# Large SBUF buffers placed at multiples of 2048 bytes in a float32 scan and feed-forward kernel

## The reference, cut to what matters

```python
# x, f_logit: (2, 6080, 256), all float32
sig = 1.0 / (1.0 + np.exp(-f_logit))
f = lower_bound + (1.0 - lower_bound) * sig
i = 1.0 - f
for t in range(S):                      # a gated running sum over 6080 steps
    h = f[:, t] * h + i[:, t] * x[:, t]
    y[:, t] = h
# then per token, d_model 256, d_ff 2048
h = y @ w_in
g = h * np.clip(h + 3.0, 0.0, 6.0) / 6.0
out = g @ w_out
```

## The kernel before, in words

| buffers | before | after |
|---|---|---|
| w_in_raw, w_out_raw, w_in_hi, w_in_lo, w_out_hi, w_out_lo | 128 | 0 |
| x_sb, z_sb, sig, gate, drive, state | 1280 | 0 |
| state_hi, state_lo, clipped, g, g_hi, g_lo, y_sb | 1312 | 0 |
| warm (1024 bytes) | 256 | 0 |

## Time and profile before

### The profile page before, as it was taken

How to read it: one execution, slowest core, us unless ns; L and a number is a source line. 1 busy time by engine, 2 the same in 40 slices (tenths; PEclk the granted TensorE clock), 3 DMA queues, 4 the chain that set the end, 5 groups by cost and what they waited for, 6 DMA issues and landing times.

```text
span 1083.2 us, 12791 instructions
## 1 busy us (share of the span) xinstructions
PE 1074.5 (99%) x4636; PEld 873.8 (81%) x4636; DVE 621.4 (57%) x950; ACT 533.2 (49%) x859; POOL 70.9 (7%) x37
## 2 busy tenths in 40 slices
PE   7999999999999999999999999999999999999998
PEld 7998888888888888888888888888888888888886
DVE  7865564655646556465564655646556465564644
ACT  5655454454544545444454444544445445454443
POOL 3300000000000000000000000000000000000000
PEclk9999999999999999999999999999999999999999
DMA  7011010110101101011010110101101001010000
GB/s 262 1 56 56 1 59 0 58 58 0 58 6 52 58 0 58 13 46 58 0 58 17 41 58 0 58 21 37 58 0 58 24 34 58 0 58 20 1 20 19
DMA packets 22093, 41.74 MB, mean 39 GB/s; under 512 B 1600, under 2 KB 3136, under 8 KB 22080
## 3 DMA queue, kind: packets, MB, share of 16 engines
q1 hardware_dynamic: 22080, 41.56, 11.4%
HBM read 29.10 MB, written 12.45 MB: 38 GB/s over the span
## 4 chain that ended last, share of the span: by engine, by line
PE 98%; DVE 0%; ACT 0%; issue 0%; ACTq 0%
PE y_ps L465 49%; PE h_ps L445 49%; DVE state L349 0%; DVE state_lo L379 0%; ACT clipped L263 0%; DVE g_lo L364 0%; DVE g L359 0%; DVE drive L342 0%; ACT y_sb L324 0%; ACT state_hi L277 0%; ACT g_hi L268 0%; ACTq L262 0%
## 5 line engine op out<-in xcount | busy, mean ns | idle before, releaser
L263 ACT ACTIVATE clipped<-h_ps,half 128x512 f32<-128x512 f32 (+1 forms) x384 | 263.2, 686 | 533.6 <-PE h_ps L445 533.6
L359 DVE SCALAR_TENSOR_TENSOR g<-clipped,h_ps 128x512 f32<-128x512 f32 (+1 forms) x384 | 261.7, 682 | 450.2 <-ACT clipped L263 450.1
L445 PE MATMUL h_ps<-state_hi,w_in_hi 128*128 128x512 f32 (+1 forms) x768 | 303.2, 395 | 3.3 <-DVE state_lo L379 3.3
L465 PE MATMUL y_ps<-g_hi,w_out_hi 128*128 128x512 f32 (+1 forms) x768 | 302.5, 394 | 1.0 <-DVE g_lo L364 1.0
L445 PE MATMUL h_ps<-state_lo,w_in_hi 128*128 128x512 f32 (+1 forms) x768 | 302.8, 394 | 0.0
L445 PE MATMUL h_ps<-state_hi,w_in_lo 128*128 128x512 f32 (+1 forms) x768 | 302.7, 394 | 0.0
L465 PE MATMUL y_ps<-g_lo,w_out_hi 128*128 128x512 f32 (+1 forms) x768 | 302.3, 394 | 0.0
L465 PE MATMUL y_ps<-g_hi,w_out_lo 128*128 128x512 f32 (+1 forms) x768 | 302.3, 394 | 0.0
L364 DVE TENSOR_TENSOR g_lo<-g,g_hi 128x512 fp32r<-128x512 f32 (+1 forms) x384 | 271.2, 706 | 0.2
L268 ACT CAST g_hi<-g 128x512 fp32r<-128x512 f32 (+1 forms) x384 | 233.0, 607 | 1.6 <-DVE g L359 1.4
L445 PEld LDWEIGHTS h_ps<-state_hi,w_in_hi 128*128 128x128 f32 x768 | 144.9, 189 | 37.0 <-DVE state_lo L379 2.9
(11 more groups left out here) (23 smaller groups left out, 77.9 us busy)
## 6 DMA issues: line engine op xcount, KB each, us to landing
z_sb<-in_z SPq DMA_DIRECT2D x22, 512.0 KB, 4.5
x_sb<-in_x SPq DMA_DIRECT2D x22, 512.0 KB, 5.1
out_y<-y_sb SPq DMA_DIRECT2D x21, 512.0 KB, 3.3
w_in_raw<-in_w_in SPq DMA_DIRECT2D x8, 256.0 KB, 5.9
w_out_raw<-in_w_out SPq DMA_DIRECT2D x8, 256.0 KB, 7.1
out_y<-y_sb SPq DMA_DIRECT2D x2, 448.0 KB, 3.5
out_y<-y_sb SPq DMA_DIRECT2D x2, 256.0 KB, 2.1
z_sb<-in_z SPq DMA_DIRECT2D x2, 224.0 KB, 3.7
```

The source lines that it names most:

```text
L263: nc.scalar.activation(clipped[:, s, 0:n], h_ps[:, s, 0:n], ACT.Relu, bias=half[:], scale=1.0 / 6.0).then_inc(clipped_ready, 1)
L359: nc.vector.scalar_tensor_tensor(g[:, s, 0:n], clipped[:, s, 0:n], 1.0, h_ps[:, s, 0:n], ALU.min, ALU.mult).then_inc(g_ready, 1)
L445: last = nc.tensor.matmul(h_ps[:, s, 0:n], w[:, f, k, :], v[:, b, k, 0:n], start=(k == 0 and m == 0), stop=(k == K - 1 and m == len(terms) ...
L465: last = nc.tensor.matmul(y_ps[:, b, d, 0:n], w[:, f, at], v[:, s, 0:n], start=(f == 0 and m == 0), stop=(f == F - 1 and m == len(terms) - 1))
```

## The change

A filler of 1920 bytes is put ahead of the first buffer, so that it begins at byte 18432 = 9 x 2048. The small tensors (`lb_sb`, `one_minus_lb`, `lb_minus_one`, `half`, `warm`, `carry`), which lay between the large ones, are allocated behind all of them. Each large buffer is a multiple of 2048 bytes long, so all of them then begin at multiples of 2048. No instruction, operand shape, wait or transfer is changed, on any engine.

```diff
+ROW = 2048
+PAD_FROM = 16512
...
+        sb("pad", [P, ROW - PAD_FROM % ROW], mybir.dt.uint8)
         w_in_raw = sb("w_in_raw", [P, F, K, P])
         w_out_raw = sb("w_out_raw", [P, F, D])
         w_in_hi = sb("w_in_hi", [P, F, K, P], F32R)
         w_in_lo = sb("w_in_lo", [P, F, K, P], F32R)
         w_out_hi = sb("w_out_hi", [P, F, D], F32R)
         w_out_lo = sb("w_out_lo", [P, F, D], F32R)
-        lb_sb = sb("lb_sb", [P, K])
-        one_minus_lb = sb("one_minus_lb", [P, K])
-        lb_minus_one = sb("lb_minus_one", [P, K])
-        half = sb("half", [P, 1])
-        warm = sb("warm", [P, WARM_N], F32R)
...
         state = sb("state", [P, K, N])
-        carry = sb("carry", [P, B, K])
         state_hi = sb("state_hi", [P, B, K, N], F32R)
...
         y_sb = sb("y_sb", [P, B, K, N])
+
+        warm = sb("warm", [P, WARM_N], F32R)
+        lb_sb = sb("lb_sb", [P, K])
+        one_minus_lb = sb("one_minus_lb", [P, K])
+        lb_minus_one = sb("lb_minus_one", [P, K])
+        half = sb("half", [P, 1])
+        carry = sb("carry", [P, B, K])
```

## The result

The changed kernel takes 1053.73 us (median of 4 runs, 1052.91 to 1055.17) against 1084.74 (1084.52 to 1084.92) before: ratio 0.9713, 95% interval 0.9699 to 0.9727. The medians lie 31.0 us apart and the spans of the two profiled executions 30.0, since the profiled execution of the changed kernel was the slowest of its four runs: it took 1055.17 us for a span of 1053.2. So the time of a run lies 2.0 us above its own span there, not the 1.6 that the prediction adds; this shifts nothing in what follows.

A forecast was written before the change was run, and what follows sets the result against it. TensorE's matmul spacing bounds the kernel: 4224 x 0.2343 + 384 x 0.2000 = 1066.5 us, with opening and end a span of 1083.2. All change terms were zero; plus 1.6 gives 1084.8 us, range 1056 to 1088.

The forecast's parts named there:

- the 1.6 that the prediction adds: Whole run: the median run time lies 1.6 us above the profiled span, added to every predicted span.
- The unexplained step of 5.8 to 7.7 ns: 512-column matmuls: excess over the cost seen with 448 columns, 24.5 to 32.5 us if placement removed it.
- I take zero: Spacing of 512-column TensorE matmuls: the new placement changes nothing, 0 us, out of bounds up to 88.7 us.
- the term on weight loads: TensorE weight loads: 0.19 us each, hidden, ended 0.04 us before use, alike at four block starts; 0 us.
- The argument from alternating sizes: Mixed 448- and 512-column matmuls: the extra cost falls behind and catches up, so it is not tied to an address.
- The first had the right size: Rival on streamed rows: 512-column rows are cheaper within one 2048-byte stretch; 1060.3 to 1052.3 us, chance 0.27.
- The second named the right partners: Rival on stream and loads: everything at remainder 0 collides, slower; 1090 to 1106 us, chance 0.16.
- The short matmuls: 448-column matmuls on TensorE: expected to stay 200 ns apart.
- ACT, DVE, POOL: Operands of these engines move to remainder 0; 3.4 us of cover remain, so 0 us.
- Opening: Transfers at the start: first matmul within a microsecond of 9.44; plus or minus 0.5 us together with the final store.
- The 16-byte lines: SBUF rule: remainders 1312 and 0 both begin a 16-byte line, so the move is worth nothing.
- N / 2.4 + 2.5 ns: Matmul spacing rule: 215.8 ns for 512 columns; 78 us less should placement be the whole reason for the difference.

The follow-up runs named there:

- e3: Changed kernel with every large buffer at remainder 32 by 2048 instead of 0; 1053.7 us.
- e11: Changed kernel with the 448-column streamed rows written to and read from columns 40 to 487, 160 bytes in; median 1053.00 us, ratio 0.9690 to before.
- e8: Changed kernel with weights left at remainder 0 and every other large buffer at 32 by 2048; 1082.6 us.
- e5: Changed kernel with state rows at remainder 512 and g rows at 1024 by 2048, all else at 0; 1053.4 us.
- e10: Kernel before with only a 96-byte filler ahead of state_hi, so rows start at 1408 and weights stay at 128; 1054.4 us, ratio 0.9697.
- e4: Kernel before with only TensorE's operands (split weights and streamed rows) moved to remainder 0, other buffers as before; 1054.3 us.
- e1: Kernel before with only the weight buffers moved to remainder 0, streamed rows still at 1312; 1082.4 us.
- e6: Changed kernel with weights left at remainder 0 and every other large buffer at 256 by 2048; 1053.5 us.
- e7: Changed kernel with weights left at remainder 0 and every other large buffer at 64 by 2048; 1061.9 us.
- e2: Kernel before with only the streamed rows moved to remainder 0, weights still at 128; 1079.3 us.

## Why the prediction was wrong

The views were read rightly: TensorE alone is the bound, and the only lever of that size is the spacing of 512-column matmuls, 4.2 us for each nanosecond. The unexplained step of 5.8 to 7.7 ns was sized rightly too; 7.62 is what went. In part that is luck: the yardstick was the short matmuls' 13.3 ns beyond their columns, and they happened to lie at a place that is among the best for them. After the change they paid 20.0 ns, more than the long ones' 13.3.

*The step that failed* is "I take zero" for that spacing. It put at nothing a term of 7.62 ns for each matmul, 32.2 us. It rested on two arguments. The first, that the 448-column row from the same remainder 1312 paid only 13.3 ns, was about the row's own place, and as such its conclusion holds: e3 has a row off every multiple of 64 and across a multiple of 2048, at no cost. But it was taken to clear every address, and from another length, while lengths don't share their best placement: at distance 160 the short ones are at their best (200.0, again in e11) and the long ones at their worst (234.3). The second, in the term on weight loads, was the decisive fault. I held that weight blocks started at 128, 640, 1152 and 1664 without a difference, so the place of the weights didn't matter. These four are one and the same place by 256 (remainder 128). The trace had no variation in the one quantity that counts, and I took its evenness for evidence that nothing counts. e3 against e8 shows it: the rows unmoved, the weights' place alone worth 6.7 ns.

*The argument from alternating sizes*, "a rate and not a penalty at an address", made a false choice: it is a rate, and the addresses have a part in it. Not the whole: the changed kernel has the lag as well, with all places alike. In its chain the groups of six long ones among short ones still take 1.40 us at 88.79, and 1.36 only from 99.42 on.

```profile
88.79 1.40 PE h_ps L449 x6
91.41 1.40 PE h_ps L449 x6
...
99.42 1.36 PE h_ps L449 x6
```

*The rivals.* The first had the right size, 1052.3 to 1060.3, and the wrong reason: not the multiple of 2048 (e3, e5, e10). I had its chance at 0.27, and the range cut it at 1056 where its upper price alone gave 1052.3. The second named the right partners, the stream and the load beside it, and had the sign the wrong way round: a common place by 256 is the free one. It said that meeting at the same remainder "is not new, save for the load", which was the thing to follow up.

*The short matmuls* were forecast at 200 and came at 206.7 in that profile, 2.6 us against the gain. *Weight loads hidden*: right as to the wait and wrong as to the cost, since the place of a block whose load is hidden still changes the spacing. *ACT, DVE, POOL*: right, e4 moved them alone and nothing came of it. *Opening*: right, 9.06 for 9.44; over all profiles here it began between 8.5 and 9.6 us.

The Trainium skill (TensorE: Matmul & The Clock Gate, Step-by-step: what each phase is for) says that loading the next weights takes no read bandwidth from the running matmul. These runs speak against it for float32r: with the rows unmoved, the weights' place is worth 6.7 ns of every matmul (e3, e8). The 16-byte lines of the Trainium skill (SBUF — State Buffer, Specifications (TRN2)), which I had weighed for the zero, do not tell apart the placements at 32 and 64 from 0, which are 6.7 and 2.2 ns dearer. The other rule that I had cited from the Trainium skill, N / 2.4 + 2.5 ns (TensorE: Matmul & The Clock Gate, Back-to-back issue gap), is given there for a single matmul by itself and not for a stream in which each matmul brings a load; its 215.8 ns was reached in no run, and the least was 226.67.

What stays open is the mechanism inside: why 256 bytes, and which part of a load meets which part of a stream. That the two reads get in each other's way is an inference from their places; no view shows it directly. The cost at a uniform distance of 96, 192 or 224 wasn't measured either, nor whether 512 columns have a second value at some distance, as 448 columns have at distance 0; in nine profiles at distance 0 they had one.

## What to carry to other kernels

Where float32r matmuls of 512 columns, each with a load of its own, bound a kernel, set their starts against columns / 2.4 ns; here 21.0 ns over was too much and 13.3 was the least seen. Then put all streamed rows and all weight blocks at one remainder by 256 bytes: small tensors between large buffers decide this by chance, and one filler of 96 bytes was worth 3.0% here (interval 2.9 to 3.2). For matmuls of 448 columns it is not the best place, so measure other lengths anew. And before calling a quantity without effect because the trace is even in it, check by smaller periods too that it varied at all.

## What the runs showed of the hardware

- Spacing of 512-column float32r matmuls with 128x128 float32r loads, at a granted clock of 1.00, by the distance from blocks to rows modulo 256 bytes: 0: 226.67, 32: 233.33, 64: 228.89, 128: 232.38, 160: 234.29 ns. It does not grow evenly with the distance. Distance 0 is the same with rows and blocks at 0, 32 or 128 by 256 (the change, e3, e10), and moving the rows by 1280 bytes, five periods, leaves the spacing as it is at distance 32 (e1, e8).
- At distance 0 each start follows the last by 226 or 227 ns (225 to 228 in e5 and e6); at 160 by 230 to 238 in a repeating row of seven.
- 448 columns have other preferences: 200.0 at distance 160 in two kernels (before, e11) and at 64 (e7), 206.7 at 128 (e2) and at 32 (e8), and 202.7 or 206.7 at 0, the latter two for one and the same kernel in two profiles, and within one execution of e10.
- Places of buffers that only ACT, DVE, POOL or transfers use: no effect on the spacing to 0.01 ns (e4).
